# Scores of the first half-sequences for two heads in one matmul, and the weight split divided anew over the engines, in a fused attention + two-MLP kernel on one Trainium2 core

## The reference

```python
scores = scale * q @ k.T + bias      # bias -slope*|rel|, mask 0 <= rel < 128
attn = softmax(scores); x = attn @ v          # heads side by side: x is (4, 576, 512)
xn = (x - mean) / sqrt(var + 1e-6) * g_ln
x = x + relu(xn @ w_ch1) @ w_ch2              # w_ch1 512x2048, w_ch2 2048x512
h = relu(x @ w_in)                            # 512x1024
conv = sum over 3 taps of conv_w[k] * h shifted by k - 1
out = (h * sigmoid(conv)) @ w_out             # 1024x512
```

## Time and profile before

| | us |
|---|---|
| median of 3 runs (797.63 to 798.58) | 798.57 |
| the profiled execution | 799.17 |
| its span, first to last instruction | 797.4 |
| TensorE busy | 782.7 |
| VectorE busy | 511.5 |
| ScalarE busy | 371.5 |
| GpSimd busy | 172.5 |

### The profile page before, as it was taken

How to read it: one execution, slowest core, us unless ns; L and a number is a source line. 1 busy time by engine, 2 the same in 40 slices (tenths; PEclk the granted TensorE clock), 3 DMA queues, 4 the chain that set the end, 5 groups by cost and what they waited for, 6 DMA issues and landing times.

```text
span 797.4 us, 17024 instructions
## 1 busy us (share of the span) xinstructions
PE 782.7 (98%) x5809; PEld 753.8 (95%) x5809; DVE 511.5 (64%) x1419; ACT 371.5 (47%) x1033; POOL 172.5 (22%) x166
## 2 busy tenths in 40 slices
PE   9989999999999999999999999999999999999998
PEld 6679889999999999989999999999998999999998
DVE  5775778764677776456776645222259888778862
ACT  7783576551355564125565422123244444444432
POOL 6676572110111211011121100111110111011100
PEclk9999999999999999999999999999999999999999
DMA  7763521301312130131213012303220211222001
GB/s 185 185 178 104 162 75 38 105 8 61 105 31 76 45 99 9 61 108 31 76 38 105 9 61 89 114 1 102 88 90 12 87 41 65 82 82 82 22 23 46
DMA packets 56494, 59.42 MB, mean 75 GB/s; under 512 B 25184, under 2 KB 43616, under 8 KB 55904
## 3 DMA queue, kind: packets, MB, share of 16 engines
q1 hardware_dynamic: 56416, 58.43, 24.2%
HBM read 44.25 MB, written 14.16 MB: 73 GB/s over the span
## 4 chain that ended last, share of the span: by engine, by line
PE 75%; issue 11%; DVE 7%; ACT 3%; POOL 3%; POOLq 0%; ACTq 0%; DVEq 0%
PE bank L1383 21%; PE bank L1385 20%; PE bank L1384 20%; PE bank L1322 3%; PE bank L1354 3%; PE bank L1336 2%; PE bank L1281 2%; PE bank L1307 2%; DVE prob L1034 1%; ACT prob L810 1%; PE bank L1294 1%; POOL small L689 1%; PE bank L1270 1%; POOL k_lo L679 1%; DVE q_st L1121 1%
## 5 line engine op out<-in xcount | busy, mean ns | idle before, releaser
L1383 PE MATMUL bank<-xn_hi,wa_hi 128*128 128x288 f32 x512 | 156.1, 305 | 1.4 <-issue 1.4
L1383 PE MATMUL bank<-h_hi,wb_hi 128*128 128x288 f32 x512 | 156.1, 305 | 0.5 <-DVE ch_stage L1102 0.5
L1384 PE MATMUL bank<-xn_lo,wa_hi 128*128 128x288 f32 x512 | 151.7, 296 | 0.0
L1385 PE MATMUL bank<-xn_hi,wa_lo 128*128 128x288 f32 x512 | 151.6, 296 | 0.0
L1384 PE MATMUL bank<-h_lo,wb_hi 128*128 128x288 f32 x512 | 150.8, 295 | 0.0
L1385 PE MATMUL bank<-h_hi,wb_lo 128*128 128x288 f32 x512 | 150.6, 294 | 0.0
L840 ACT ACTIVATE h_hi<-bank 128x288 fp32r<-128x288 f32 x128 | 52.4, 409 | 175.3 <-PE bank L1385 174.2
L1091 DVE SCALAR_TENSOR_TENSOR h_lo<-bank,h_hi 128x288 fp32r<-128x288 f32 x128 | 58.2, 455 | 112.6 <-ACT h_hi L840 110.9
L1383 PEld LDWEIGHTS bank<-xn_hi,wa_hi 128*128 128x128 f32 x512 | 96.5, 188 | 2.9 <-issue 2.0
L1383 PEld LDWEIGHTS bank<-h_hi,wb_hi 128*128 128x128 f32 x512 | 96.3, 188 | 2.5 <-issue 1.2
L1384 PEld LDWEIGHTS bank<-xn_lo,wa_hi 128*128 128x128 f32 x512 | 96.6, 189 | 0.0
(11 more groups left out here) (133 smaller groups left out, 1671.3 us busy)
## 6 DMA issues: line engine op xcount, KB each, us to landing
k_raw<-qkT SPq DMA_DIRECT2D x48, 144.0 KB, 2.8
q_raw<-qkT SPq DMA_DIRECT2D x48, 144.0 KB, 2.9
x_in<-x_spill SPq DMA_DIRECT2D x8, 580.0 KB, 4.1
ch_in<-ch_spill SPq DMA_DIRECT2D x8, 580.0 KB, 5.1
x_spill<-xT SPq DMA_DIRECT2D x4, 1152.0 KB, 4.2
ch_spill<-ch_stage SPq DMA_DIRECT2D x32, 144.0 KB, 1.9
out<-out_stage SPq DMA_DIRECT2D x32, 144.0 KB, 1.8
wa_raw<-w SPq DMA_DIRECT2D x16, 256.0 KB, 3.5
```

Of the source, the lines that this page charges most:

```text
L1383: nc.tensor.matmul(dst, w_h, a_h, start=start, stop=False)
L1384: nc.tensor.matmul(dst, w_h, a_l, start=False, stop=False)
L1385: last = nc.tensor.matmul(dst, w_l, a_h, start=False, stop=stop)
```

## The change

1. **Scores in pairs.** One matmul makes a score tile of two heads: the queries of the even head stand in rows 0 to 63 and those of the odd head in rows 64 to 127 of the stationary operand, the keys of each in its own column block with zeros in the other rows. The columns streamed are as many as before, the weight loads half. There are two buffers (pairs), not four (heads); each tile has a bank of its own. `HS` items exist for even heads only.
2. **WARM** has 5 matmuls instead of 10.
3. **Weights.** `w1` is loaded in its natural layout, so that the gain is a column over partitions; ACT applies it as it makes `hi` (`scale=`), DVE as it makes `lo` (one scalar_tensor_tensor). `w_gain` is gone. GpSimd makes both `hi` and `lo` of `w2`. A hidden tile needs four `w1` tiles now. Six `w1` and twelve `w2` tiles are split in the prologue, ten and four in "first".
4. All eight `half_pt` copies of c=1 are ACT's.
5. **Late weights.** Tiles of `w_in`, `w_out` come in another order, 1.5 slots apart from slot 38.5 instead of 2 from slot 33; the last four of `w_out` lie in `wb_lo`.

```diff
-HALF_PROLOGUE = {("HS", 0): -0.3, ("HS", 1): -0.28, ("HP", 0): 1.8, ("HO", 0): 2.75}
+HALF_PROLOGUE = {("HX", 0): -0.3, ("HP", 0): 1.8, ("HO", 0): 2.75}
+PAIR_SCORES = (-0.3, -0.29, -1.0)
-WARM = [(1.79, 10)]
+WARM = [(1.79, 5)]
...
+W1_PROLOGUE, W1_FIRST = [2.1, 3.1, 4.1, 5.1, 6.1, 7.1], [0.25, 2.05, 3.85, 5.65, 7.45, 9.25, 11.05, 12.85, 14.65, 16.45]
+W2_PROLOGUE, W2_FIRST = [3.0, 4.0, 5.0, 6.0, 7.0, 8.0, 9.2, 10.15, 11.1, 12.05, 13.0, 13.95], [-0.6, 0.6, 1.6, 16.2]
...
 def half_items(c, start, slots, at, heads):
-    return [(start + slots * h + t, (kind, c, h, x)) for h in heads for (kind, x), t in at.items()
-            if kind != "HS" or x < len(HGROUPS[c])]
+    pairs = [(start + slots * h + (PAIR_SCORES[x] if c or h else PAIR_SCORES[0] + 0.01 * x), ("HS", c, h, x))
+             for h in heads if h % 2 == 0 for x in range(HNT[c])]
+    return pairs + [(start + slots * h + t, (kind, c, h, x)) for h in heads for (kind, x), t in at.items()]
...
-        out += [(2 * (F1 + m) + 1, ("W", NW1 + m)) for m in range(NW2)]
+        out += [(38.5 + 1.5 * i, ("W", NW1 + i)) for i in range(NW2)]
...
-            return c == 1 and 1 <= h <= 5
+            return c == 1
...
+        def hi_by_pool(n):
+            return n < NW1 and not first_layer(n)
+        def lo_by_pool(n):
+            return not first_layer(n) if n < NW1 else n % 2 == 1
...
-                nc.gpsimd.tensor_tensor(kc, kc, g_col[:].unsqueeze(2).broadcast_to((P, DC, P)), ALU.mult).then_inc(w_prep, 1)
...
-                nc.scalar.activation(w_tile(n)[1], w_raw(n), ACT.Copy).then_inc(w_hi_ready, 1)
+                nc.scalar.activation(w_tile(n)[1], w_raw(n), ACT.Copy, scale=gain(n) if first_layer(n) else 1.0).then_inc(w_hi_ready, 1)
...
+                if first_layer(n):
+                    nc.vector.scalar_tensor_tensor(lo, w_raw(n), gain(n), hi.bitcast(F32), ALU.mult, ALU.subtract).then_inc(w_split_dve, 1)
...
             def half_scores(c, h, x):
...
+                qk = half_qk[e // 2 % 2]
+                for i in (e, e + 1):
+                    pe.wait_ge(half_qk_loaded[i % 4], 16 * (i // 4 + 1))
...
+                nc.tensor.matmul(dst[0:rows, 0:2 * keys].rearrange("p (h k) -> p h k", h=2), qk[:, 0, q0:q0 + rows],
+                                 qk[:, 1:3, k0:k0 + keys], start=True, stop=True).then_inc(bank_filled, 1)
```

More of the change, by code:

```diff
@@ L137, with last_step @@
 NORM_ORDER = [x[0::2] for _, x in sorted(norm_items(0, 0))]
+LATE_TILES = [0, 1, 12, 2, 3, 13, 4, 5, 14, 6, 7, 15, 8, 9, 10, 11]
+IN_WA = 12
+assert sorted(LATE_TILES) == list(range(NW2))
+def last_step(m):
+    return m // DC * DC + DC - 1
 def is_int(batch):
@@ L166, in timeline @@
         out += [(t, ("WARM", n)) for t, n in WARM]
-        out += [(t, ("W", n)) for n, t in enumerate(W_TIMES)]
+        out += [(t, ("W", n)) for n, (first, t, _) in enumerate(W_TIMES) if not first]
         return sorted(out, key=lambda x: x[0])
@@ L170, in timeline @@
     if kind == "first":
-        out += [(0.25 + W_PACE * (n - W_PROLOGUE), ("W", n)) for n in range(W_PROLOGUE, NW1)]
+        out += [(t, ("W", n)) for n, (first, t, _) in enumerate(W_TIMES) if first]
         out += HALF_FIRST
@@ L297, in build @@
         half_pt0 = sb("half_pt0", [P, 512], scope=half)
-        half_qk2 = sb("half_qk2", [P, 2, 384], scope=half)
+        half_v = [sb(f"half_v{i}", [P, 3, D], scope=half) for i in range(4)]
         half_pt1 = sb("half_pt1", [P, 512], scope=half)
-        half_qk3 = sb("half_qk3", [P, 2, 384], scope=half)
+        sb("half_gap0", [P, 4 * 3 * D], scope=half)
         sb("half_gap1", [P, 2 * S + NT * D], scope=half)
@@ L315, in build @@
         half_pt = [half_pt0, half_pt1]
[L316 to L317 removed]
+        assert PTN - 512 == 4 * 3 * D and 3 * 384 == DC * CH
         half.close()
@@ L893, in run @@
                         evacuate(batch, a[0])
-                    elif name == "w" and a[0] not in W_HI_POOL:
+                    elif name == "w" and not hi_by_pool(a[0]):
                         w_hi(*a)
@@ L974, in half_minima @@
                 dve.nop(nofuse=True)
-                for t, at in HGROUPS[c][x]:
+                for t in range(HNT[c]):
                     rows, _, _, keys, b0, col = HTILES[c][t]
                     r = half_rows(c, h) + t
+                    item = ("HS", c, h - h % 2, t)
+                    src = bank[bank_of(0, item)][0:rows, keys * (h % 2):keys * (h % 2) + keys]
+                    dve.wait_ge(bank_filled, use_of(0, item) + 1)
+                    dve.nop(nofuse=True)
                     ins = nc.vector.tensor_tensor_reduce(
-                        out=half_prob_of(c, h)[0:rows, col:col + keys], in0=src[0:rows, at:at + keys],
+                        out=half_prob_of(c, h)[0:rows, col:col + keys], in0=src,
                         in1=half_dist[0:rows, h, b0:b0 + keys], scale=-SCALE, scalar=BIG, op0=ALU.add, op1=ALU.min,
@@ L1157, in run @@
                         evacuate(batch, a[0])
-                    elif name == "w" and not by_pool(a[0]):
+                    elif name == "w" and not lo_by_pool(a[0]):
                         w_lo(*a)
@@ L1476, in result @@
                 last = product(out_bank[d % 2][:, 0:CH],
-                               [(wa_hi[:, F2 + f, P * d:P * (d + 1)], wa_lo[:, F2 + f, P * d:P * (d + 1)], g_hi[:, c, f, :],
-                                 g_lo[:, c, f, :], f == 0, f == F2 - 1) for f in range(half * part, half * (part + 1))])
+                               [(*w_out_part(f, d), g_hi[:, c, f, :], g_lo[:, c, f, :], f == 0, f == F2 - 1)
+                                for f in range(half * part, half * (part + 1))])
                 if part == 1:
```

176 lines of the change are left out of this document (87 added, 89 removed).

## The result

The changed kernel takes 806.22 us (median of 4; 804.53 to 809.82) against 798.52; the ratio is 1.0104, with a 95% interval of 1.0089 to 1.0119. It is slower by 1.0%, where I had forecast 0.25% faster: both the sign and the range were wrong. The profiled execution took 804.53 us, its span 802.7 (before: 799.17 and 797.4).

The account below looks back on a forecast made before the run. TensorE, busy 782.7 of 797.4 us, was taken to bound the kernel. +0.4 up to "first" and -2.5 in it gave -2.1, a span of 795.3 and a forecast of 796.6 us (-0.25%), range 794.0 to 800.0.

Parts of the forecast that it names:

- Part 1: Prologue's beginning: second pair waits for the fourth head's load, landing at 9.1; first transposes at 12.5 instead of 12.09, +0.4 us.
- Part 2: Prologue scores: a pair takes 2.2 us against 2.64 in c=0, and 1.83 against 1.94 in c=1.
- pairs bring nothing: Rival on the prologue scores: 2.5 us a pair, +1.0, 797.5 us; within the range, no separate chance.
- Part 3: Prologue, c=0: TensorE idles 0.85 us for the copy before outputs of heads 0, 2, 4, 6; +3.4 us.
- Part 4: Prologue: VectorE gets six `w_lo`, mean about 1.05 us each; its slot of 3.4 is just covered by TensorE's 3.5.
- the 0.3: Microseconds added in the prologue for VectorE's six `w_lo`, whose time was just covered by TensorE's.
- VectorE paces the prologue: Rival: each of six `w_lo` waits out a GpSimd `lo`, 2.0 us, delaying outputs; 800 to 801 us; chance 0.2.
- Part 5: From c=0's end (39.35) to "first": 14.2 us of work plus 2.0 of waits; "first" begins at 55.85, +0.4.
- Part 6: In "first": VectorE's load stays the same but delays leave the softmax chain; -2.5 us, bounds 0 and -3.9.
- the sign of being wrong: Prediction's sign called wrong if "first" begins after 58 or TensorE's waits in "first" do not shrink.
- cancelled: Rival: ten `w_lo` in the softmax chains of "first" cost what GpSimd cost; -0.5 there, sum 0, 798.5 us; chance 0.15.
- part 7: Late weights: ready before the second MLP needs them, now and later, with TensorE busy throughout; 0 us.

Follow-up runs that it names:

- part D: Third score tile of each pair moved between even head's transposes and outputs, on cured kernels (800.12, 797.60): 819.13 us; with minima and exponentials behind the copy, 818.82.

## Why the prediction was wrong

- **Part 1, the start: right in its mechanism, mis-sized.** The second pair does wait for head 3's load. I let it land 4.1 us after its issue, by the earlier trace rows; it took 4.4, and up to 0.9 more elsewhere. The first transposes stood at 12.76, not 12.5, and at up to 15.25 in other runs. I gave the term no range; what it lacked is that the same wait can lower the clock.
- **Part 2, pairs:** 2.18 and 1.82 against 2.2 and 1.83. Right, and "pairs bring nothing" is out.
- **Part 3, the stall of the even heads:** 0.88 us four times, 3.5 in the waits list, against 3.4. From 12.76 to 39.58 are 26.82 us; I had 26.85.
- **Part 4:** `w_lo` took 735 to 874 ns in the prologue, 774 in the mean, against 1.05 us; the 0.3 did not come. The rival "VectorE paces the prologue", my only way to a slower kernel, did not happen: three of the six began while GpSimd was at work, with 0.2 to 0.35 us of its instruction left (746, 803 and 874 ns). The one at 90.98 began with 0.85 left and took 1.39 us. By the Trainium skill's rule on two-input VectorE instructions against GpSimd (SBUF — State Buffer, Who interferes with whom), a `w_lo` waits for the rest of what GpSimd has begun; the trace agrees, each being lengthened by what was left less 0.2 us or so. What I had wrong is how much of it is left when a `w_lo` starts.
- **Part 5:** the wait of 1.3 for `first_x_tok` became 0.4, others of 0.4 and 0.5 came. From 39.58 to 56.71 are 17.1 us; I had 14.2 and 2.0 of waits: 0.9 too little. The scores took 1.25 us less than before (I had 1.2) and the waits 0.84 less (I had 1.0); what I left out is that the transposes around the normalisation took 0.6 us longer, why is open. "First" began at 56.71, not 55.85.
- **Part 6 is the step that failed by its mechanism.** I wrote that "the delays go from the chain of a head's softmax to places between", and took 2.5 us for it. Ten positions in the table decide that, and I did not hold them against VectorE's order. Two of them are in front of `pt_lo`. It gave 0.2, and the waits in "first" did not shrink, which I had named as the sign of being wrong. Rival "cancelled" described it, at 0.15.
- **Missing altogether, and the largest part of the miss:** the position of TensorE's code. It cost 3.8 us by medians (806.2 against 802.4) and 5.1 at the edge in the profiled run (2.7 of stall, 2.4 of clock). The prediction put all that stands behind "first" at 0 (part 7) and did not name the 1.2 us of "issue" at 342, which can grow. No term of a sum over instructions can show it, but the count of instructions ahead of the loop could have: 45 pairs of weight load and matmul fewer.

In spans the miss is 7.4 us (802.7 against 795.3): 0.9 up to "first", 2.3 in it, 0.5 in the first steady batch and 5.1 at the edge, less 1.4 regained behind it. Without the code's position I would still have been wrong by 5.8 us (802.4 against 796.6): the start and part 5 ("first" began 0.9 to 3.3 us late), part 6 (2.3 us and more) and small waits in the first steady batch (0.5 to 1.3).

What stays open: why the clock fell behind waits of 1.24 and 1.84 us in two runs and held behind 2.76 in another; and ScalarE's stall, as said.

## What to carry to other kernels

Before a small difference is put down to an edit, look at every loop's back edge in both traces: an edit far ahead moves the loop's head within its block of code, and one extra matmul, or a hint on the branch, tells whether 3 us and the clock behind them are the edit's. When work is moved to another engine, write out that engine's order around each thing that the bound engine waits for; the sum of its load says nothing on the chain. When two pieces of work become one, its inputs are needed earlier: move their loads first. And when a cure is found on the way, give it to the kernel before as well, before the change is judged by it.

## What the runs showed of the hardware

- The taken branch at the end of the steady loop (some 2,280 recorded instructions on TensorE) took 3.3 to 3.6 us there (4.4 once); with the hint 0.39 in the changed kernels and 2.50 in the kernel before the change. A second stall behind it showed as 2.7 to 3.2 us. The second MLP's loop, of some 800, took its branch in 0.22 to 0.24 us.
- In all three profiled kernels with the second stall (2.67 and 3.21 us; 3.91 in one piece with the first) the clock fell inside it and stayed at 1.2 GHz for 6.83 us; each matmul of 288 columns took its turn in 0.24 us there instead of 0.133. Waits of 1.24 to 2.27 us came with 3.41 us of it in six places (part D aside); other waits, of 1.20, 1.7, 2.60 and 2.76 us, with none.
- A `w_lo` on VectorE took 0.73 to 0.75 us when GpSimd was idle, and up to 1.39 us when it began behind a GpSimd instruction under way.
